# A pass in front of TensorE's attention loop in which a test of the loop counter skips every part, and nine zero products ahead of it in place of three

## The reference

```python
def _attn_ref(q, k, v, mem_k, mem_v):          # 4 x 8 heads x 768 x 64
    for c in range(nc):                        # chunks of 32
        k_full = np.concatenate([mem_k, k[:, :, l_start:r_end]], axis=2)
        scores = scale * np.matmul(q_c, k_full.transpose(0, 1, 3, 2))
        a = np.exp(scores - np.max(scores, axis=-1, keepdims=True))
        a = a / (np.sum(a, axis=-1, keepdims=True) + 1e-09)
        out[:, :, c_start:c_end] = np.matmul(a, v_full)
...
    logits = x @ w_gate                        # x: 3072 x 512
...
        h = np.maximum(x[mask] @ w1[e], 0.0)   # each expert, 384 tokens
        out[mask] = h @ w2[e]
...
    h = x @ w_in
    solu = h * softmax(h)
    return (ln(solu) * g_ln) @ w_out
```

## Time and profile before

| | us |
|---|---|
| median of 3 runs (lowest, highest) | 759.92 (757.53, 759.92) |
| the profiled execution | 760.91 |
| its span | 759.1 |
| TensorE busy, of the span | 705.1 (93%) |
| VectorE, ScalarE, GpSimd busy | 528.4, 328.0, 321.4 |
| mean granted TensorE clock | 0.948 of 2.4 GHz |

### The profile page before, as it was taken

How to read it: one execution, slowest core, us unless ns; L and a number is a source line. 1 busy time by engine, 2 the same in 40 slices (tenths; PEclk the granted TensorE clock), 3 DMA queues, 4 the chain that set the end, 5 groups by cost and what they waited for, 6 DMA issues and landing times.

```text
span 759.1 us, 17892 instructions
## 1 busy us (share of the span) xinstructions
PE 705.1 (93%) x7122; PEld 626.4 (83%) x7122; DVE 528.4 (70%) x1918; ACT 328.0 (43%) x537; POOL 321.4 (42%) x242
## 2 busy tenths in 40 slices
PE   7899993299999999999999999999999999999992
PEld 5788883289888989898989898889888988899882
DVE  4366757788888788868886888688778877542240
ACT  1255556242465146414741474157315722571360
POOL 2011105684375156515751574167317731762011
PEclk8599995599999999999999999999999999999997
DMA  8689997350331032103321331132113301330001
GB/s 341 209 307 371 386 339 277 97 167 2 98 112 55 29 123 100 65 26 120 104 77 33 106 113 56 55 98 98 56 57 112 111 30 56 111 111 29 1 15 41
DMA packets 24925, 89.09 MB, mean 117 GB/s; under 512 B 3360, under 2 KB 3360, under 8 KB 24864
## 3 DMA queue, kind: packets, MB, share of 16 engines
q0 software_dynamic: 13056, 46.14, 18.7%
q1 hardware_dynamic: 11808, 42.17, 15.0%
HBM read 75.71 MB, written 12.58 MB: 116 GB/s over the span
## 4 chain that ended last, share of the span: by engine, by line
PE 86%; DVE 9%; issue 2%; ACT 1%; POOL 0%; DVEq 0%; POOLq 0%
PE banks L563 24%; PE banks L565 22%; PE banks L564 22%; PE banks L486 3%; PE banks L443 3%; PE banks L467 3%; PE banks L592 2%; PE bank L453 2%; PE bank L478 2%; DVE inv L1228 2%; PE banks L576 1%; DVE ul L1252 1%; DVE flips L1060 1%; PE bank L556 1%; PE bank L505 1%
## 5 line engine op out<-in xcount | busy, mean ns | idle before, releaser
L1413 POOL TENSOR_TENSOR wl<-raw,wh 128x1024 fp32r<-128x1024 f32 x60 | 146.6, 2444 | 30.6 <-ACT wh L780 29.4
L1407 POOL DMA_INDIRECT raw<-w,w_idx x60 | 67.3, 1121 | 151.8 <-DVE w_idx L1123 110.8
L563 PE MATMUL banks<-xh,wh 128*128 128x384 f32 x256 | 90.2, 352 | 2.2 <-DVE xl L1259 2.2
L563 PE MATMUL banks<-hh,wh 128*128 128x384 f32 x256 | 90.2, 353 | 0.0
L565 PE MATMUL banks<-xh,wl 128*128 128x384 f32 x256 | 86.3, 337 | 0.0
L565 PE MATMUL banks<-hh,wl 128*128 128x384 f32 x256 | 86.3, 337 | 0.0
L564 PE MATMUL banks<-xl,wh 128*128 128x384 f32 x256 | 85.9, 336 | 0.0
L564 PE MATMUL banks<-hl,wh 128*128 128x384 f32 x256 | 85.9, 335 | 0.0
L563 PE MATMUL banks<-wout_h,uh 128*128 128x512 f32 x192 | 79.1, 412 | 0.0
L563 PE MATMUL banks<-win_h,yh 128*128 128x512 f32 x192 | 77.4, 403 | 0.0
L565 PE MATMUL banks<-wout_h,ul 128*128 128x512 f32 x192 | 75.4, 393 | 0.0
(11 more groups left out here) (202 smaller groups left out, 1573.7 us busy)
## 6 DMA issues: line engine op xcount, KB each, us to landing
unit<-qk_in SPq DMA_DIRECT2D x24, 768.0 KB, 6.3
vr<-v_in SPq DMA_DIRECT2D x24, 520.0 KB, 5.1
x_rows<-x_keep SPq DMA_DIRECT2D x20, 256.0 KB, 5.2
prep_first<-w_in SPq DMA_DIRECT2D x4, 512.0 KB, 7.1
x_rows<-x_sb SPq DMA_DIRECT2D x4, 256.0 KB, 4.5
prep_first<-w_out SPq DMA_DIRECT2D x2, 512.0 KB, 9.0
prep_rest<-w_out SPq DMA_DIRECT2D x2, 512.0 KB, 10.2
raw<-w,w_idx POOLq DMA_INDIRECT x60, 4.3
```

The source lines that it names most:

```text
L563: nc.tensor.matmul(bank, stat_h, mov_h, start=first, stop=False)
L1407: gp.indirect_dma_start(stage(s, c), None, table, bass.IndirectOffsetOnAxis(ap=w_idx[:, c % WCH:c % WCH + 1], axis=0))\
L1413: gp.tensor_tensor(wl[:, c % WCH, :], stage(s, c), wh[:, c % WCH, :].bitcast(F32), ALU.subtract)\
```

## The change

The loop gets one pass more, counted from 0 to 6 in place of 0 to 5. Its four steps are cut into six parts, and each stands behind `pe.If(b > 0)`, so that in the pass with b = 0 every part is jumped over. The pieces keep their order: scores, probs_T, gate, x_T, values; the last three that are neither scores nor values are now in `between`. Unit numbers are counted from `b * DEEP - DEEP`. A threshold must be positive for every value of the register, so the constants of the zero fillings grow; VectorE's fillings are the same operations with other counts. The zero products ahead of the loop go from three to nine.

```diff
@@ -49,9 +49,9 @@
 DEEP = 4
 RING = DEEP * CPT
 KEPT = NT - DEEP
-BLANK_PT, BLANK_X, BLANK_XT, BLANK_SHIFTED, BLANK_GATE = 2, 2, 3, 2, 4
+BLANK_PT, BLANK_X, BLANK_XT, BLANK_SHIFTED, BLANK_GATE, BLANK_PROBS = 6, 6, 7, 6, 8, 5
 TG = 12
-WARM = 3
+WARM = 9
 G = E * TG
 NEG = -1.0e38
 MARK = 1000.0
@@ -447,7 +447,7 @@
 
             def probs_T(i, r):
 
-                pe.wait_ge(probs, i + 1)
+                pe.wait_ge(probs, i + BLANK_PROBS)
                 pe.wait_ge(pT_sb, i - 1 + BLANK_PT)
                 for hp in range(HP):
                     mm = nc.tensor.transpose(PT_PS[:, hp * P:(hp + 1) * P],
@@ -486,30 +486,38 @@
                     mm = nc.tensor.matmul(GATE_PS[r % 2], xT[:, r % 2, k, :], wg[:, k, :], start=(k == 0), stop=(k == KD - 1))
                 mm.then_inc(gate_ps, 1)
 
-            def step(i, r, n):
+            def between(i, r):
 
                 known = isinstance(i, int)
-                if not known or i < NT:
-                    scores(i, r, n)
                 if not known or i <= NT:
                     probs_T(i, (r - 1) % DEEP)
                 gate(i, (r - 3) % DEEP)
                 if not known or i <= NT + 1:
                     x_T(i, (r - 2) % DEEP)
-                if not known or i <= NT:
-                    values(i, (r - 1) % DEEP, n)
-
-            pe.wait_ge(probs, 1)
+
+            pe.wait_ge(probs, BLANK_PROBS)
             blank = pr[:, 1, :, :, :].rearrange("p h a w -> p (h a w)")
             for _ in range(WARM):
                 nc.tensor.matmul(PT_PS[:, :], blank[:, 0:P], blank, start=True, stop=True)
             pe.wait_ge(consts, 1)
             pe.wait_ge(small_in, 32)
-            with pe.Fori(0, NT // DEEP) as b:
-                for r in range(DEEP):
-                    step(b * DEEP + r, r, b + 1)
+            with pe.Fori(0, NT // DEEP + 1) as b:
+
+                for pair in range(0, DEEP, 2):
+                    i, j = b * DEEP + (pair - DEEP), b * DEEP + (pair + 1 - DEEP)
+                    with pe.If(b > 0):
+                        scores(i, pair, b)
+                        between(i, pair)
+                    with pe.If(b > 0):
+                        values(i, (pair - 1) % DEEP, b)
+                        scores(j, pair + 1, b)
+                    with pe.If(b > 0):
+                        between(j, pair + 1)
+                        values(j, pair, b)
             for i in range(NT, NT + 3):
-                step(i, i % DEEP, NT // DEEP + 1)
+                between(i, i % DEEP)
+                if i == NT:
+                    values(i, (i - 1) % DEEP, NT // DEEP + 1)
 
 
             def best_T(f):
@@ -932,12 +940,12 @@
         @block.vector
         def _(ve):
             ve.sem_inc(shifted, BLANK_SHIFTED)
-            nc.vector.memset(pr[:, 1, :, :, :], 0.0).then_inc(probs, 1)
-            nc.vector.memset(xT[:, 1, :, :], 0.0).then_inc(xT_sb, 1)
-            nc.vector.memset(x_sb[:, 2, :, :, :], 0.0).then_inc(x_ready, 1)
+            nc.vector.memset(pr[:, 1, :, :, :], 0.0).then_inc(probs, BLANK_PROBS)
+            nc.vector.memset(xT[:, 1, :, :], 0.0).then_inc(xT_sb, BLANK_XT - 2)
+            nc.vector.memset(x_sb[:, 2, :, :, :], 0.0).then_inc(x_ready, BLANK_X - 1)
             nc.vector.memset(pT[:, :, :, :], 0.0).then_inc(pT_sb, BLANK_PT)
             nc.vector.memset(vr[:, RING - CPT:RING, :, :], 0.0).then_inc(v_loaded[DEEP - 1], 16)
-            nc.vector.memset(xT[:, 0, :, :], 0.0).then_inc(xT_sb, BLANK_XT - 1)
+            nc.vector.memset(xT[:, 0, :, :], 0.0).then_inc(xT_sb, 2)
             nc.vector.memset(x_sb[:, 3, :, :, :], 0.0).then_inc(x_ready, 1)
 
             def soften(u, r, masks):
```

## The result

| | before | after |
|---|---|---|
| median of 4 runs each, us (lowest, highest) | 759.76 (757.53, 759.92) | 770.47 (768.86, 771.35) |
| the profiled execution, us | 760.91 | 771.35 |
| its span, us | 759.1 | 769.6 |
| TensorE busy, us (of the span) | 705.1 (93%) | 708.2 (92%) |
| mean granted TensorE clock, of 2.4 GHz | 0.948 | 0.950 |

The ratio is 1.0147, 95% interval 1.012 to 1.0173: slower by 10.7 us, where 16.6 us were forecast. The sign and the mechanism came out as forecast, the size at 0.64 of it, inside the range.

A forecast was written before the change was run, and what follows sets the result against it. It blamed instruction-fetch stalls in the loop's first pass and the low clock. Start 26.2 + steps 84.9 + tests 7.2 + clock 5.3 = loop end 123.6 us, not 106.99: +16.6, forecast 776.5 us, range 757 to 787.

The forecast's parts named there:

- Four fetches one after the other: Pass in front: blocks 2 to 5 each fetched on demand, times adding up; first score product at 26.2 us, not 7.04.
- The price of a miss: Pass in front: 6.0 us for block 2, 5.2 for block 3, 4.2 each for blocks 4 and 5.
- the least busy case: Block 5's fetch in the kernel before: asked for at 28.09 us, packet at 29.9, taken as 4.2 us.
- The tests: Compare-and-branch, branch and register instructions around the loop's six parts: 7.2 us in all, bounds 2.4 and 14.6.
- The idle pieces that I had announced: Sign to look for in the loop: TensorE idle for 0.2 to 0.5 us at each second step.
- 0.115 each, in full: Price per test instruction, from the old branch back: 4 instructions costing 0.46 us.
- The clock: Loop start: idle TensorE from 12.1 to 26.2 us drops it to 1.2 GHz for 13.2 us, costing 5.3 us.
- Behind the loop: After the last gate product nothing changes; all of it shifts by the same time as the loop's end.
- The fetches are hidden: Rival for the pass in front: all four fetches end under the zero products, 757.2 us; chance 0.20.
- the limit: Price of one miss at which the hidden-fetch rival breaks even: loop start at 14.9 us, 2.1 us per block.
- Two at a time: Rival for the pass in front: a missing block's neighbour is fetched too, start at 17.3 us, 766.0 us; chance 0.15.
- The loop no longer stays loaded: Rival for the loop: a seventh block pushes out block 0, each branch back misses, 802 us; chance 0.05.

The follow-up runs named there:

- early16: Changed kernel with the waits for constants and small loads moved from before the loop into its first part, and 16 zero products: 772.98 us, ratio 1.0174.
- quiet_after: Changed kernel with only units 0 and 1 and the first vr loaded ahead, other loads held until the first scores ran: 765.96 us, ratio 1.0095.
- The variant that starts at 18.04 us: Changed kernel with the waits moved into the loop, nine zero products and later loads held until the first scores ran: 763.35 us, ratio 1.0051.

## Why the prediction was right in kind and too large

**Four fetches one after the other: right.** The packets came in the order forecast, the last one needed at 21.7 us (forecast: behind 20). They lay 5.1, 3.2 and 3.0 us apart, where I had written over 4, and over the 2.5 that would have spoken against me. The first was at 10.3 us, each jump went on 2.3 to 2.5 us behind its packet, and TensorE was idle from 12.41 to 25.01 us. Removing one miss (three zero products) moved the start by 3.15 us, one bare miss.

**The price of a miss: too high, by 2.6 us in the sum.** "Block 2 6.0, block 3 5.2, blocks 4 and 5 4.2 each", 19.6 us, were 6.15, 4.84, 3.08 and 2.96, 17.0. The first two were near. The step that failed is the least busy case: between 28.09 us, when block 5 was asked for, and its packet at 29.94 the DMA engines moved 255 GB/s, and 4.2 us was not the bare price. Where the loads had landed or were held back it was 2.8 to 3.5 us in every kernel, mostly 3.0: the packet came 0.4 to 1.2 us behind the jump, and not 1.85. Against this, entering the loop and the branches that find their code took 25.01 - 6.1 - 17.0 = 1.9 us where I put 0.5. The start is off by only 1.2 us, 25.0 against 26.2, because these two errors partly cancel; that is luck.

**The tests: the term that failed most.** Forecast 7.2 us, measured 0.56 us a pass in the changed kernel, 3.4 us in six, and 3.4 us with the tests alone in the kernel. By their places, in the changed kernel: from the top of a pass to its third step are 51.64 - 44.52 = 7.12 us (66.36 - 59.22 = 7.14 in the next), where two bare steps of 3.42 are 6.84, so the tests there cost 0.28 to 0.30, not 0.65; from there to the next top 59.22 - 51.64 = 7.58, two bare steps and a branch back 7.30: 0.28, not 0.54. The idle pieces that I had announced, 0.2 to 0.5 us at each second step, are 0.15 or none at the third step and 0.59 at the top, where 0.37 was there before. The step that failed was "0.115 each, in full", taken from the branch back. That branch *jumps*, and a jump that finds its code takes 0.21 to 0.23 us by itself; a test that falls through takes 0.07, and the branch behind a part, which goes to the next instruction, has no row in the trace: its price was not measured apart, but with the register instructions it is within the 0.56 us of a pass. A taken branch and one that isn't are two prices, and I had a row for one. By the Trainium skill ("Advanced Engine Details and Errata", Control Flow Timing) a compare-and-branch takes about 108 ns; the 68 ns and 0.22 us here lie on either side of it, and the sum that I had set beside mine by it, some 2 us less, was nearer and still too high.

**The clock: right in kind; in size, luck.** 13.01 us at 0.50 (13.2 forecast), 4.8 us lost (5.3 forecast). Part of the 0.5 us between is a misread row. I took 39.62, where a piece of the chain begins, for the start of the next step; the timeline has it at 39.41:

```profile
39.41 1.17 PE L443 MATMUL banks<-unit 64*32 64x64 f32 x64
```

So a slow step is 39.41 - 33.83 = 5.58 us, 2.16 more than a fast one and not 2.37, and 2.3 of them are 5.0 us (the product as I wrote it, 2.3 x 2.37, would be 5.5). And that the low clock would last as long behind the start as it had in an unbroken stretch before is not what the other kernels show. In two of them, with three zero products and with 16 (`early16`), idle for 15.57 and 9.84 us before the start, it lasted half as long:

```profile
21.86:29.22 7.36, 7.36 (x211) 6.69 (x212) 2.12 (x4) 0.63 (x1) 0.00 (x0) 0.50 0.09 18
28.52:35.12 6.60, 6.60 (x208) 6.01 (x208) 1.55 (x3) 0.63 (x1) 0.00 (x0) 0.50 0.00 0
```

Over all eight kernels with a pass in front that lost the clock it was 6.6 to 13.0 us behind the start, near 7 in four and above 12 in four. The first pass took from 38.86 - 21.69 = 17.17 us (`quiet_after`) to the 19.51 of the changed kernel, so the term was worth 2.5 to 4.8 us. No run shows what decides it; that the forecast met it is luck.

**Behind the loop: right.** 10.46 us there, 10.5 in the span.

The sum with what was measured: 25.0, plus 24 x 3.42 and five branches back of 0.46 (84.4; I had counted six, but behind the last pass there is none), plus 0.56 x 6 = 3.4, plus 4.8, is 117.6 us. The trace has 117.45. Of the 6.0 us between this sum and mine, the tests are 3.8, the start 1.2, the sixth branch back and the clock 0.5 each. (The tests' terms add up to 7.14 us as they stand, not 7.2; this changes nothing.)

**The rivals.** *The fetches are hidden* is out: the limit was 2.1 us a block, and with hardly any load a miss costs 2.8 at the least. The limit itself, a start at 14.9 us with the clock kept, was too strict: with the measured tests it is 106.99 - 84.4 - 3.4 = 19.2 us, or (19.2 - 6.1 - 1.9) / 4 = 2.8 us a block, the price of the cheapest miss. The variant that starts at 18.04 us is ahead of it and still 3.2 us slower than the kernel before, since it lost the clock. *Two at a time* is out: every packet came behind the jump that wanted it. *The loop no longer stays loaded* is out: no packet from 25 to 120 us with seven blocks loaded, six of which the loop runs. The 128 KB in lines of 16 KB that the Trainium skill gives ("Advanced Engine Details and Errata", ISA Cache) fit this; its two lines don't.

**Left open.** Why the first miss stays at 4.75 to 5.23 us where the later loads are held back: its packet came behind the first three loads (342 and 299 GB/s until then), and it took 3.39 us when it ran at 17.7 us, but no run takes those three away. What decides how long the low clock lasts, and which pacing is the best one. Held clock and the best start were not run together: 18.04 + (115.55 - 24.98) = 108.6 us would be the loop's end with the zero products in the jumps, an estimate from two kernels, and behind 106.99. If the clock were kept without those parts, it would be 18.04 + 84.4 + 3.4 = 105.8 us, 1.2 us ahead of 106.99; no run has that either.

## What to carry to other kernels

To run over code once without executing it does not preload it for free: a jump into a block that isn't loaded has nothing to hide it, and four of them in a row cost more than the stalls that they were to remove, which had products running beside most of the fetch. First relieve the transfers that share the DMA engines with the instruction fetches: two transfers in flight rather than seven gained 0.96% here (0.9904, 0.9881 to 0.9927), for five waits. And where the program's start is bound by code, count instructions: 24 more of them in front moved one test over a block's edge and cost 3.15 us.

## What the runs showed of the hardware that was not expected

- **A fetch's price hangs on the data in flight.** A jump into a missing block of 256 instructions took 2.8 to 3.5 us with the DMA engines near idle (5 to 27 GB/s), 5.8 to 6.6 us with them full (385 to 420 GB/s). From packet to first instruction it was 2.3 to 2.8 us throughout; the rest is the wait for the packet, 0.4 to 4.3 us.
- **The sequencer ran 35 or 36 instructions ahead of these float32 products and no more.** In two kernels it reached the loop with that many instructions of zero products left, and with 36 in all it wasn't held.
- **The jump that is taken costs three times the one that isn't:** 0.21 to 0.25 us against 0.07, over all kernels. Only the first jump into block 1 took more, 0.34 to 0.36 us.
- **Zero products that run at the jumps keep the clock.** 28 rows in 12.28 us of misses were enough for 1.00 throughout, and a gap of 6.00 us was enough to lose it for over 12 us. How long it stays low differs: 7.36 us behind a gap of 15.57, 12.4 behind one of 6.00.
